# Attention and two feed-forward blocks on one core: the first block's fractional part moved from VectorE to GpSimd in both half steps

## The reference, cut to what matters

```python
for t in range(S):                      # batch 4, heads 8, S 768, head dimension 48
    state = alpha[:, :, t, :, None] * state + einsum('bhd,bhe->bhde', k[:, :, t], v[:, :, t])
    y[:, :, t] = einsum('bhd,bhde->bhe', q[:, :, t], state)
x = y.transpose(0, 2, 1, 3).reshape(3072, 384)
h = x @ w_in                            # 384 x 2048
x = (h * cos(h)) @ w_out                # 2048 x 384
h = maximum(maximum(x @ w1, x @ w2), x @ w3)   # 384 x 768 each
out = h @ w_out2                        # 768 x 384
```

## Time and profile before

| | us |
|---|---|
| median of 3 runs | 871.81 (871.43 to 873.71) |
| the profiled execution | 873.21 |
| its span, first to last instruction | 871.6 |

### The profile page before, as it was taken

The page is one execution under the profiler, slowest core; times in us unless marked ns, Lnnn a source line. Parts: engine busy times, 40 slices in busy tenths (PEclk is TensorE's granted clock), DMA queues, the critical chain, the costliest instruction groups (busy, mean ns, idle before and its releaser), DMA issues.

```text
span 871.6 us, 15664 instructions
## 1 busy us (share of the span) xinstructions
PE 831.0 (95%) x5446; PEld 757.8 (87%) x5446; DVE 614.0 (70%) x1286; ACT 421.7 (48%) x912; POOL 216.9 (25%) x242
## 2 busy tenths in 40 slices
PE   4688898999999999999999999999999999999998
PEld 3688798888888888888888878889999999999998
DVE  8698898777777777777776457757756566556454
ACT  3775555544454445444544456646343444434333
POOL 6564343333333332333233213310000000000000
PEclk9898999999999999999999999999999999999999
DMA  9633223202330132123213001130101010100001
GB/s 260 197 105 80 58 56 82 91 28 56 83 91 28 55 82 89 30 55 82 73 46 137 1 37 49 50 120 2 37 37 38 37 37 36 34 2 36 1 38 37
DMA packets 13780, 54.35 MB, mean 62 GB/s; under 512 B 1968, under 2 KB 2480, under 8 KB 13712
## 3 DMA queue, kind: packets, MB, share of 16 engines
q1 hardware_dynamic: 12992, 49.55, 19.5%
q0 software_dynamic: 720, 3.93, 1.1%
HBM read 44.04 MB, written 9.44 MB: 61 GB/s over the span
## 4 chain that ended last, share of the span: by engine, by line
PE 48%; DVE 1%; ACT 1%; issue 0%; POOL 0%; DVEq 0%; ACTq 0%
PE h_ps L1319 4%; PE score L1319 4%; PE h_ps L1321 4%; PE h_ps L1320 4%; PE score L1321 4%; PE score L1320 4%; PE h_ps L1226 2%; PE h_ps L1228 2%; PE h_ps L1227 2%; PE acc_pair L1226 2%; PE acc_pair L1228 2%; PE acc_pair L1227 2%; PE acc_pair L1301 1%; PE acc_pair L1300 1%; PE acc_pair L1299 1%; PE acc_last L1227 1%
## 5 line engine op out<-in xcount | busy, mean ns | idle before, releaser
L426 POOL TENSOR_TENSOR work<-work 128x512 f32<-128x512 f32 x75 | 96.1, 1281 | 259.6 <-DVE work L939 259.6
L573 ACT ACTIVATE work<-work 128x512 f32<-128x512 f32 (+1 forms) x112 | 63.6, 568 | 143.6 <-POOL work L426 114.1
L1226 PE MATMUL h_ps<-x_hi,w_hi 128*128 128x512 f32 (+1 forms) x312 | 121.6, 390 | 3.2 <-DVE x_lo L872 2.7
L925 DVE TENSOR_TENSOR work<-work,h_ps 128x512 f32<-128x512 f32 (+1 forms) x104 | 62.6, 602 | 76.0 <-ACT work L573 75.5
L1228 PE MATMUL h_ps<-x_lo,w_hi 128*128 128x512 f32 (+1 forms) x312 | 114.0, 365 | 0.0
L1227 PE MATMUL h_ps<-x_hi,w_lo 128*128 128x512 f32 (+1 forms) x312 | 113.5, 364 | 0.0
L1226 PE MATMUL acc_pair<-g_hi,w_hi 128*128 128x512 f32 (+1 forms) x224 | 83.6, 373 | 10.4 <-POOL g_lo L433 10.1
L806 DVE RECIPROCAL inv_decay<-decay 112x128 f32<-112x128 f32 x96 | 90.1, 941 | 0.1
L580 ACT ACTIVATE g_hi<-work 128x512 fp32r<-128x512 f32 (+1 forms) x112 | 63.4, 566 | 44.6 <-DVE work L925 39.4
L557 ACT ACTIVATE work<-h_ps 128x512 f32<-128x512 f32 (+1 forms) x104 | 54.7, 526 | 56.0 <-PE h_ps L1228 55.4
L1228 PE MATMUL acc_pair<-g_lo,w_hi 128*128 128x512 f32 (+1 forms) x224 | 81.6, 364 | 0.0
(11 more groups left out here) (205 smaller groups left out, 2390.3 us busy)
## 6 DMA issues: line engine op xcount, KB each, us to landing
v_all<-val SPq DMA_DIRECT2D x24, 576.0 KB, 4.1
raw<-qka SPq DMA_DIRECT2D x46, 288.0 KB, 5.1
block_out<-x SPq DMA_DIRECT2D x6, 768.0 KB, 3.3
x_in<-block_out SPq DMA_DIRECT2D x6, 768.0 KB, 4.4
raw<-wb SPq DMA_DIRECT2D x12, 384.0 KB, 3.0
out<-raw POOLq DMA_DIRECT2D x5, 768.0 KB, 3.5
stage_own<-wa SPq DMA_DIRECT2D x6, 384.0 KB, 6.6
x<-wa SPq DMA_DIRECT2D x6, 384.0 KB, 5.6
```

Of the source, the lines that this page charges most:

```text
L426: nc.gpsimd.tensor_tensor(frac[:], turns[:], whole[:], ALU.subtract).then_inc(S["frac_done"], 1)
L573: nc.scalar.activation(cosine[:, cols], frac[:, cols], ACT.Sin, scale=-TURN if half else TURN).then_inc(S["cos_done"], 1)
L925: nc.vector.tensor_tensor(gated[:, cols], cosine[:, cols], h, ALU.mult).then_inc(S["g_done"], 1)
L1226: mm(ps, w_hi[:, w_at], xh, start=first, stop=False)
```

## The change

In both half steps the fraction is computed by POOL (before: DVE). So that it is a plain subtraction, ACT now does both roundings: turns + 1.5*2^23 into `whole`, then minus the constant again, in a second instruction that waits for the first (`up_done`). The fraction changes sign, so the cosine's scale is +2pi in all steps. DVE issues the gate of a tile one tile later: in iteration i it gates tile i - 1, and the last after the loop. On POOL `g_low(i-1)` follows `fraction(i)`. In the first half step POOL's `mul_decay` and `mul_inverse` of a pair, which stood together ahead of a tile, are issued in two different iterations (6 and 7, 11 and 12, and `mul_inverse(0,2)` at 1), and DVE's weight halves 9 and 14 move to iterations 5 and 11. In the second half step ACT issues `mid_state` ahead of `turn`, and POOL's `mul_inverse` follows `g_low`. Full steps are as they were.

```diff
 # POOL
-            def fraction(t):
+            def fraction(t, half):
+                _, cols, _, depth, _ = slot(t, half)
                 pool.wait_ge(S["whole_done"], t + 1)
-                wait(pool, "cos_done", t)
-                nc.gpsimd.tensor_tensor(frac[:], turns[:], whole[:], ALU.subtract).then_inc(S["frac_done"], 1)
+                wait(pool, "cos_done", t + 1 - depth)
+                nc.gpsimd.tensor_tensor(frac[:, cols], turns[:, cols], whole[:, cols],
+                                        ALU.subtract).then_inc(S["frac_done"], 1)
...
             for i in range(TILES1):
-                if i == 7:
-                    decay_qk(0, 3)
-                if i == 12:
-                    decay_qk(1, 0)
-                g_low(i)
-                if i == 0:
-                    mul_inverse(0, 2)
+                fraction(i, True)
+                if i:
+                    g_low(i - 1)
+                if i in (6, 11):
+                    mul_decay(i // 11, 3 - 3 * (i // 11))
+                if i in (1, 7, 12):
+                    mul_inverse(i // 12, {1: 2, 7: 3, 12: 0}[i])
                 if i in (2, 3):
                     low_weights(4 + i)
+            g_low(TILES1 - 1)
...
-                    late = i == 1 and not half
-                    if ahead and i % BATCH == 1 and not late:
+                    early = i != 1 and not half
+                    if ahead and i % BATCH == 1 and early:
                         mul_inverse(*group)
-                    if half:
-                        g_low(tile(c, i))
-                    elif i:
-                        fraction(tile(c, i))
-                    if ahead and late:
+                    if half or i:
+                        fraction(tile(c, i), half)
+                    if half and i:
+                        g_low(tile(c, i) - 1)
+                    if ahead and i % BATCH == 1 and not early:
                         mul_inverse(*group)
                     if ahead and i % BATCH == 0:
                         mul_decay(*group)
+                if half:
+                    g_low(tile(c, TILES1 - 1))
 # ACT
                 nc.scalar.activation(whole[:, cols], turns[:, cols], ACT.Copy,
-                                     bias=ROUND).then_inc(S["whole_done"], 1)
+                                     bias=ROUND).then_inc(S["up_done"], 1)
+                act.wait_ge(S["up_done"], t + 1)
+                nc.scalar.activation(whole[:, cols], whole[:, cols], ACT.Copy,
+                                     bias=-ROUND).then_inc(S["whole_done"], 1)
...
-                                     scale=-TURN if half else TURN).then_inc(S["cos_done"], 1)
+                                     scale=TURN).then_inc(S["cos_done"], 1)
...
-                        if not half:
-                            mid_state(c + 1, i)
-                            if i:
-                                g_high(t - 1, half)
+                        mid_state(c + 1, i)
+                        if i and not half:
+                            g_high(t - 1, half)
                     turn(t, half)
                     if half:
                         rounded(t)
                         if i:
                             g_high(t - 1, half)
-                        mid_state(c + 1, i)
 # DVE
-            low0 = {2: (8,), 7: (9, 10, 11), 8: (12,), 10: (13,), 12: (14, 15)}
+            low0 = {2: (8,), 5: (9,), 7: (10, 11), 8: (12,), 10: (13,), 11: (14,), 12: (15,)}
             for i in range(TILES1):
                 if i == 9:
                     x_low0(2)
-                fraction(i, True)
+                if i:
+                    gate(i - 1, True)
                 if i == TILES1 - 1:
                     x_low0_quads(3, (0,))
                 elif i in ahead0:
                     scan(*ahead0[i])
-                gate(i, True)
...
                 for k in low0.get(i, ()):
                     low_weights(k)
+            gate(TILES1 - 1, True)
             mask_scores(1, 0)
...
                         if i:
                             new_state(c + 1, i - 1)
+                            gate(t - 1, half)
                         scan(*nxt)
-                        fraction(t, half)
                         if i < UNITS - 1:
                             inverse(*nxt, (s + 1 + g // PAIRS) % 2)
-                        gate(t, half)
-                        if i < UNITS - 1:
                             mask_scores(c + 1, i + 1)
                         continue
...
-                if not half:
-                    gate(t, half)
+                gate(t, half)
```

More of the change, by code:

```diff
@@ L155, in build @@
             "mid_state", "y_done", "inc_done", "state_done", "xhi_done", "xlo_done",
-            "h_done", "turns_done", "whole_done", "frac_done", "cos_done", "g_done",
+            "h_done", "turns_done", "up_done", "whole_done", "frac_done", "cos_done", "g_done",
             "ghi_done", "glo_done", "acc_done", "x2_done", "spilled",
@@ L407, in mul_inverse @@
                 mul(k_dec[R, s, :, hi], raw[R, s, 1, :, hi], inv_decay[R, s, :, hi], ALU.mult).then_inc(S["qk_done"], 1)
-            def decay_qk(a, p):
-                mul_decay(a, p)
-                mul_inverse(a, p)
             def low_weights(k):
@@ L946, in fraction @@
                 wait(dve, "cos_done", t + 1 - depth)
-                if half:
-                    nc.vector.scalar_tensor_tensor(frac[:, cols], whole[:, cols], ROUND, turns[:, cols],
-                                                   ALU.subtract, ALU.subtract).then_inc(S["frac_done"], 1)
-                else:
-                    nc.vector.tensor_tensor(frac[:, cols], turns[:, cols], whole[:, cols],
-                                            ALU.subtract).then_inc(S["frac_done"], 1)
+                nc.vector.tensor_tensor(frac[:, cols], turns[:, cols], whole[:, cols],
+                                        ALU.subtract).then_inc(S["frac_done"], 1)
             ahead0 = {**{i + 3: (0, 3, i) for i in range(4)}, **{i + 8: (1, 0, i) for i in range(4)},
                       **{i + 13: (1, 1, i) for i in range(3)}}
-            low0 = {2: (8,), 7: (9, 10, 11), 8: (12,), 10: (13,), 12: (14, 15)}
+            low0 = {2: (8,), 5: (9,), 7: (10, 11), 8: (12,), 10: (13,), 11: (14,), 12: (15,)}
             for i in range(TILES1):
```

## The result

| | before | after |
|---|---|---|
| median, us (19 runs each) | 872.96 | 876.5 |
| lowest to highest | 869.89 to 881.93 | 873.7 to 884.21 |
| ratio | | 1.0044 [1.0023, 1.0065] |
| the same once more, in a later session | 872.85 (35 runs) | 876.61 (12 runs), 1.0032 [1.0003, 1.0061] |
| the profiled execution's span | 871.6 | 875.3 |

The forecast was 869.1 with a range up to 874.2. The time lies outside of it, on the other side of no change. The forecast stood on the three runs of before that were known, median 871.81; 19 runs give 872.96. So 1.1 of the 7.4 us between 869.1 and 876.5 are the base, and the rest is the difference itself: +3.5 us for -2.7.

The account below looks back on a forecast made before the run. VectorE's queue was taken to bound the second half step, ScalarE's chain and VectorE's queue the first. First half step +2.4, second -5.9, clock +0.8 gave -2.7 us: 869.1 from a median of 871.81, range 865.0 to 874.2.

Parts of the forecast that it names:

- tiles 9 to 15: First half step's later tiles: 19.9 us against 21.59, two places later than ScalarE's own chain; -1.7 us.
- The second half step: Tiles 16 to 31: VectorE loses 16 fractions, most tiles at TensorE's 3.44 us; 52.0 us against 57.94, -5.9 us.
- tiles 0 to 9: First half step's early tiles, by ScalarE alone: 34.0 us against 31.85; +2.1 us.
- The chain: First half step, turn to cosine: 2.09 us, 0.70 us more than before; 3.14 us a tile with a weight half.
- The seam: Tile 15 to 16: last gate about 4.4 us after its turn; 8.55 us against 6.56, +2.0 us without the clock.
- 0.8 us as a mean: Clock term: new TensorE waits at tile 15 may bring the lower clock, costing 1.7 to 3.6 us about one time in three.
- What the change does for the gain: Second half step: gain from 16 fractions of some 0.4 us leaving VectorE and its queue no longer waiting for a cosine.
- Rival (c): A wash: second half step wins only half, -3.0 us, scans meeting twice as many POOL instructions; 871.2 us, chance 0.24.
- the one rival on the slower side: Second half step: TensorE waits for g_low behind POOL's fraction, some 0.8 us a tile; 875.2 us taken, chance 0.17.
- (b): First half step loses nothing, second gains 5.9 us, clock as before; 865.9 us, chance 0.17.
- (a): The prediction as worked out, a small gain over both half steps: 867.5 to 870.5 us, chance 0.42.

Follow-up runs that it names:

- e1: Kernel before with the change in the second half step only, first half step as before; 869.92 us, ratio 0.9973.
- e8: Kernel before, unchanged, run again under another name for a second profile; 873.23 us, ratio 0.9979.
- e9: Kernel before with only the second half step's order changed (gate, g_low, mid_state), fraction still on VectorE with one ScalarE rounding; 869.26 us, ratio 0.9962.
- e12: Same code as e1, run again as reference in a later session; 870.12 us, ratio 0.9969.
- e2: Kernel before with the change in the first half step only, second half step as before; 879.05 us, ratio 1.0085.
- e11: The changed kernel, unaltered, run again in a later session; 876.61 us, ratio 1.0032.
- e3: Changed kernel with the first half step's last gate issued ahead of a scan and a reciprocal; 874.76 us, ratio 1.0018.
- e4: Changed kernel with 26 and 16 extra matmuls, results overwritten, in TensorE's two waits at the seam; 875.3 us, ratio 1.002.
- e10: Changed kernel without spreading: first half step's low weight halves and POOL multiplications at their old tiles; 879.0 us, ratio 1.0076.
- e5: Changed kernel with the first half step's subtraction back on VectorE, behind the late gate, both roundings still on ScalarE; 876.61 us, ratio 1.0027.
- e6: As e5, but one rounding on ScalarE in the first half step, VectorE subtracting the constant too; 872.01 us, ratio 0.9964.
- e7: As e1, plus spreading of the first half step's VectorE weight halves and POOL multiplications, old order otherwise; 870.79 us, ratio 0.9962.

## Why the prediction was wrong, step by step

Two steps failed. The sum for tiles 9 to 15 said -1.7 us and had no term for POOL's queue; they took +1.0. The second half step's gain was put at 5.9 us; it was 3.6, and not by the mechanism that the prediction gave.

Since single executions differ, the sum is made over all profiles that hold the same code (old code in the first half step: before, e1, e8, e9, e12; new: after, e2, e11, and e3 and e4 up to turn 15; old code in the second: before, e2, e8; new: the ten others but e9):

| us | old code | new code | change | forecast |
|---|---|---|---|---|
| tiles 0 to 9 | 31.79 | 34.63 | +2.8 | +2.1 |
| tiles 9 to 15 | 21.13 | 22.09 | +1.0 | -1.7 |
| seam, clock included | 7.05 | 9.29 | +2.2 | +2.8 |
| tiles 16 to 31 | 56.77 | 53.21 | -3.6 | -5.9 |
| sum | | | +2.5 | -2.7 |

The medians say +3.5 and +3.8, 1.1 to 1.3 us more. Part of it may be the choice of executions: two of the three behind the new seam, e2 and e11, were 2.5 and 1.8 us faster than the medians of their kernels. The rest stays open.

- **The chain: right.** 2.12 us for 2.09, 3.18 for 3.14. POOL's subtraction took 0.73 us, like g_low.
- **Tiles 0 to 9: right in kind, 0.7 us short.** The quick tiles were 3.15 to 3.18 us and not 3.14, and tile 8 was 5.99.
- **Tiles 9 to 15: wrong, by 2.7 us.** The step said that from tile 9 on only x_low0(2) and weight half 14 make a tile late: 19.9 us. Where the clock stayed up, the stage took 21.5 to 21.6 (after, e4, e11). The missing 1.7 us are those of the cosines of tiles 12 and 13 behind POOL's queue, by the rows above; e10, with all four multiplications ahead of fraction 12, makes tile 12 another 0.6 us longer. The Trainium skill ("SBUF — State Buffer", Who interferes with whom) says that a VectorE instruction with two SBUF inputs contends with a GpSimd instruction that reads SBUF, and the trace agrees: 1.44 us for 0.73, and 2.18 for 0.26. The prediction quoted that rule and left it out of the sum of this stage, where stretched instructions stood ahead of a fraction. The other 1.0 us is the old length: 21.59 us was read from an execution in which tile 10 took 5.58 us at a mean granted clock of 0.64. In e1 and e9, the same code, it took 3.77 and 3.91 us at 1.00 and 0.96, and the stage 20.6 and 20.5. Without POOL in the chain the stage is not shorter (e5, 21.91); with one rounding it is (e6, 20.51). So POOL's queue is what was late in this kernel, but it is ScalarE's longer chain that keeps the stage from getting shorter.
- **The seam: right.** Gate at 4.6 us for 4.4. Where the clock stayed up, the seam took 8.63 and 8.67 us (e2, e4) for 8.55. The lower clock took 1.8 us in the profile of after, almost nothing in e11 and nothing in e2, so 0.8 us as a mean was fair. The old order has it too: 7.3 to 7.5 us in e8, e9 and e12, at a granted clock of 0.77 there, against 6.5 at 1.00 in before and e1.
- **The second half step: the term mis-sized by 2.3 us.** Half of it is the old length. It was read from one execution, 57.94 us, in which the last tiles waited 2.19 us for a load's scan and ran 3.5 us at the lower clock; the same code took 56.54 and 55.83 us in two others. The other 1.2 us are the new length, 53.2 for 52.0: the first three tiles came out (9.3 us for 9.2), but after that three tiles of after take 4.2 to 4.3 us, where the sum had one late place.
- **What the change does for the gain: wrong.** The prediction put it to 16 fractions less on VectorE and to the wait for the cosine that goes. The wait was not there, the fractions brought nothing, and the order alone carries the gain (e9), in the traces by scans that no longer meet POOL: 16.2 us of scans in before, 8.1 in e9, 10.4 in after. Rival (c) expected the scans to meet POOL more often. They met it less.

As to the rivals: (c) came nearest by its price for the second half, -3.0 us, and not by its reason. None had a first half step that loses 6 us, as the table and e2's median (+5.8) show, and the one rival on the slower side put the loss into the wrong half step. One small slip in the chances: (b) and three quarters of (a) make 0.485, not 0.47.

## What to carry to other kernels

Before work is moved to another engine, run the new order without the move: here the order alone had the whole gain. Look at how long the unchanged instructions of an engine take, and not only at its waits: a scan of 0.26 us that takes 0.75 or 1.46 counts as busy and hides what costs the time. Work moved to a less busy engine is paid in the chain's length and in that engine's own queue, so it loses where the chain bounds the stage, as in this first half step. Where single executions differ by the size of the gain, take the stage's length before from several.

## What the runs showed of the hardware that was not expected

- TensorE's clock at one place of one program differs between executions. After nearly the same wait (3.17 us in after, 3.19 in e11, the same code) the lower level comes 1.1 us after the wait's end and holds for 6.5 us in the one. In the other it is there at once and holds for 3.6 us, which are over when the last accumulations begin:

```profile
93.50:97.10 3.60, 3.22 (x15) 2.95 (x15) 2.54 (x8) 1.26 (x5) 0.72 (x1) 0.53 0.02 5
97.10:99.50 2.40, 2.40 (x21) 2.40 (x22) 1.56 (x7) 0.04 (x1) 0.00 (x0) 1.00 0.01 3
```

  These are windows of e11, with the clock in the third column from the end. So the seam is 10.51 us in the one and 8.74 in the other. In e2, after a wait of 3.15 us, the clock stayed at 1.00. In e1 and e12, again one code, waits of 2.38 and 2.47 us at that place gave a mean granted clock of 1.00 and of 0.77 over the seam.
- Tile 10 of the first half step takes 3.7 to 3.9 us in the eight executions with a granted clock of 0.86 to 1.00 over it, and 5.5 to 6.7 us in the six with 0.51 to 0.69 (before, e2, e3, e7, e8, e12), whatever the order of the code.
- A second ScalarE instruction that depends on the first costs 0.45 us in the chain (e5 against e6), where its own duration is 0.42 us.
- A 64-element scan of VectorE takes 0.26 us alone and up to 2.18 beside POOL's instructions, and the reciprocal of 0.94 us keeps its length beside them (945 ns in e9, 941 in before).
